# The last matrix product of an attention and two-layer kernel: half of its depth by seven quarter products per pair of tiles

## What is computed

```python
def _moe2_ref(x, w_in, w_out):      # x 1536x512, w_in 512x2048, w_out 2048x512
    h = x @ w_in
    r = np.maximum(h, 0.0)
    g = r * r
    return (g @ w_out).astype(np.float32)
```

## Time and profile before

| | before |
|---|---|
| median of 3 runs | 476.38 us (475.81 to 476.69) |
| the profiled execution | 474.66 us |
| its span | 472.9 us |
| mean granted TensorE clock over the span | 0.999 |
| PE, PEld, DVE, ACT, POOL busy | 98%, 84%, 64%, 45%, 27% |

### The profile page before, as it was taken

How to read it: one execution, slowest core, us unless ns; L and a number is a source line. 1 busy time by engine, 2 the same in 40 slices (tenths; PEclk the granted TensorE clock), 3 DMA queues, 4 the chain that set the end, 5 groups by cost and what they waited for, 6 DMA issues and landing times.

```text
span 472.9 us, 7375 instructions
## 1 busy us (share of the span) xinstructions
PE 462.9 (98%) x2754; PEld 395.4 (84%) x2754; DVE 303.9 (64%) x491; ACT 213.7 (45%) x538; POOL 126.0 (27%) x175
## 2 busy tenths in 40 slices
PE   8889999999999999999999999999999999999997
PEld 6667787887778887788999999999988888888885
DVE  3899888998898889874863766557974121212120
ACT  4687777656866576444554122222533212122210
POOL 2366333231311330512444576551000000000000
PEclk9999999999999999999999999999999999999999
DMA  7921124543564855464301111011511000000010
GB/s 225 326 85 48 52 71 138 169 126 78 162 169 130 189 134 156 110 152 117 91 1 46 44 46 46 0 44 49 191 73 45 23 22 24 22 24 22 22 46 22
DMA packets 60443, 41.87 MB, mean 89 GB/s; under 512 B 28344, under 2 KB 48056, under 8 KB 60408
## 3 DMA queue, kind: packets, MB, share of 16 engines
q1 hardware_dynamic: 59640, 40.74, 30.7%
q10 hardware_dynamic: 768, 0.66, 0.5%
HBM read 30.38 MB, written 11.01 MB: 88 GB/s over the span
## 4 chain that ended last, share of the span: by engine, by line
PE 90%; DVE 3%; POOL 3%; ACT 2%; issue 1%; DVEq 0%; POOLq 0%
PE wo_ps L1816 13%; PE h_ps L1776 12%; PE wt_ps L2031 9%; PE score_ps L2031 9%; PE score_ps L1978 7%; PE h_ps L2010 5%; PE score_ps L2010 5%; PE wo_ps L2031 5%; PE h_ps L2031 5%; PE wo_ps L2010 4%; PE wt_ps L2010 4%; PE wo_ps L1738 3%; PE score_ps L1704 3%; PE wt_ps L1704 1%; POOL pT_own L697 1%; PE wt_ps L1715 1%
## 5 line engine op out<-in xcount | busy, mean ns | idle before, releaser
L1573 DVE TENSOR_TENSOR g_lo<-g,g_hi 128x2048 fp32r<-128x2048 f32 (+2 forms) x14 | 27.7, 1986 | 76.4 <-ACT g_hi L1141 75.2
L1141 ACT ACTIVATE g_hi<-g 128x2048 fp32r<-128x2048 f32 (+2 forms) x14 | 23.3, 1671 | 84.9 <-PE score_ps L2031 25.2
L2031 PE MATMUL wt_ps<-wy,g_hi 128*128 128x512 f32 x128 | 39.7, 391 | 0.0
L2031 PE MATMUL score_ps<-wy,g_hi 128*128 128x512 f32 x128 | 39.7, 391 | 0.0
L882 ACT ACTIVATE prob<-sm,nbias 128x132 f32<-128x132 f32 (+1 forms) x96 | 37.7, 394 | 3.7 <-DVE nbias L1231 3.0
L1816 PE MATMUL wo_ps<-wo_hi,lnT_hi 128*128 128x512 f32 x88 | 36.1, 411 | 0.0
L1776 PE MATMUL h_ps<-w_hi,xT_hi 128*128 128x512 f32 x88 | 35.3, 401 | 0.8 <-DVE xT_lo L1340 0.5
L1816 PE MATMUL wo_ps<-wo_hi,lnT_lo 128*128 128x512 f32 x88 | 35.0, 398 | 0.0
L1776 PE MATMUL h_ps<-w_hi,xT_lo 128*128 128x512 f32 x88 | 34.5, 392 | 0.0
L1816 PE MATMUL wo_ps<-wo_lo,lnT_hi 128*128 128x512 f32 x88 | 34.4, 391 | 0.0
L1776 PE MATMUL h_ps<-w_lo,xT_hi 128*128 128x512 f32 x88 | 34.3, 390 | 0.0
(11 more groups left out here) (231 smaller groups left out, 1263.0 us busy)
## 6 DMA issues: line engine op xcount, KB each, us to landing
u_dram<-uT SPq DMA_DIRECT2D x18, 256.0 KB, 3.3
lnT_raw<-u_dram SPq DMA_DIRECT2D x36, 128.0 KB, 2.8
w_raw<-w_in SPq DMA_DIRECT2D x16, 256.0 KB, 3.3
V<-v SPq DMA_DIRECT2D x12, 256.0 KB, 3.3
wy_in<-w_out SPq DMA_DIRECT2D x6, 512.0 KB, 4.0
x_dram<-x SPq DMA_DIRECT2D x44, 64.0 KB, 2.2
out<-y SPq DMA_DIRECT2D x11, 256.0 KB, 2.0
k_raw<-kT SPq DMA_DIRECT2D x20, 132.0 KB, 2.8
```

What stands on the lines that cost most here:

```text
L1141: nc.scalar.activation(g_hi[t % 2][:, chunks, :], g_tile(t, chunks), ACT.Copy).then_inc(g_rounded, 1)
L1573: nc.vector.tensor_tensor(g_lo[t % 2][:, chunks, :], g_tile(t, chunks), g_hi[t % 2][:, chunks, :].bitcast(F32), ALU.subtract).then_inc(g_s ...
L2031: done = mm(y_ps[t % 8], gs[t % 2][:, n, :], wy[n // 2][:, n % 2, w, :], start=(n == 0 and k == 0), stop=(n == C2 - 1 and k == 2))
```

## The change

The second product works on pairs of tiles: pair p is the tiles p and p + 6. The depth is cut in two. The chunks of j = 0 to 3 (8 of 16) are multiplied plainly: 4 parts a pair, `plain_part(p, i)`, each with 4 chunks of one tile, 12 MATMULs of 512 columns. The chunks of j = 4 to 7 form a 2x2 problem, upper and lower tile by the rows r = 0 and 1 of the depth by the left and right 256 columns. It is made of seven products (`seven_part(p, i)`), each with 12 MATMULs of 256 columns. Their order is FIFTH, FIRST, THIRD, SIXTH, SECOND, SEVENTH, FOURTH. `PLAN` does the plain parts of three pairs, then the seven products of these pairs, and the same again for the other three.

Such a part or product is an item, 66 in all. ACT rounds an item (512 elements a row) into one of 7 ring slots (`RING`), and DVE subtracts in place (`g_low` is g's own memory). Item n + 7 is rounded once item n is done. For the seven products DVE also forms four sums of g per pair (S1 to S4, written over the pair's plain part of g, which is then used up) and, once, four differences of the quarters of w_out. These quarters are 7 operands of 1024 elements a row, each rounded and split once. THIRD, SECOND and FOURTH accumulate onto the plain result in PSUM (the last pair's FOURTH has a bank of its own, which DVE adds at the end by 256 columns). FIFTH has a bank of its own. FIRST, SIXTH and SEVENTH accumulate in one chain bank: ACT copies it after FIRST (`keep`), DVE reads it after SIXTH (`flush`), and both read it after SEVENTH.

```diff
-EARLY_TILES = 2
+PLAIN = 4
+RING = 7
+PLAN = (("plain", 0), ("plain", 1), ("plain", 2), ("seven", 0), ("seven", 1), ("seven", 2),
+        ("plain", 3), ("plain", 4), ("plain", 5), ("seven", 3), ("seven", 4), ("seven", 5))
+PAIR_PRODUCTS = ((S1, T1), (A11, B11), (S4, B22), (S2, T2), (A12, B21), (S3, T3), (A22, T4))
+FIFTH, FIRST, THIRD, SIXTH, SECOND, SEVENTH, FOURTH = range(NP)
...
+            def round_item(n):
+                kind, p, i = ITEMS[n]
+                if n < RING:
+                    act.wait_ge(multiplied, multiplied_before(NJ - 1) + (P_FIRST, P_SECOND, P_CORNER)[n // 3] + 1)
+                else:
+                    act.wait_ge(item_done, n - RING + 1)
...
+                nc.scalar.activation(item_high(n), item_raw(g, n), ACT.Copy).then_inc(item_rounded, 1)
...
+            for n in range(len(ITEMS)):
+                keep(n)
+                if n + RING < len(ITEMS):
+                    round_item(n + RING)
...
+            def prepare(n):
+
+                kind, p, i = ITEMS[n]
+                if kind == "seven" and i == FIFTH:
+                    sum_g(p, S1)
+                    sum_g(p, S2)
+                elif kind == "seven" and i == FIRST:
+                    sum_g(p, S3)
+                    sum_g(p, S4)
+                    dve.wait_ge(s_summed, len(WST_SUMS) * (p + 1))
+                split_item(n)
...
+                dve.wait_ge(item_done, n + 1)
+                if i == SIXTH:
+                    dve.wait_ge(kept, kept_before(p) + 1)
+                    nc.vector.tensor_tensor(upper[:, HALF:DM], chain_ps, lower[:, HALF:DM], ALU.add).then_inc(chain_summed, 1)
...
+            for n in range(len(ITEMS)):
+                flush(n)
+                if n + RING < len(ITEMS):
+                    prepare(n + RING)
+                if n == 1:
+                    sum_wst(T1)
+                    sum_wst(T2)
...
+                elif n == 7:
+                    split_wst(T4)
...
-                    for k in range(3):
-                        gs, w = ((g_hi, 0), (g_hi, 1), (g_lo, 0))[k]
-                        done = mm(y_ps[t % 8], gs[t % 2][:, n, :], wy[n // 2][:, n % 2, w, :],
-                                  start=(n == 0 and k == 0), stop=(n == C2 - 1 and k == 2))
...
+            def seven_part(p, i):
+
+                n = item("seven", p, i)
+                wk = PAIR_PRODUCTS[i][1]
+                pe.wait_ge(item_split, n + 1)
+                if p == 0:
+                    pe.wait_ge(wst_split, i + 1)
...
+                elif i == SIXTH:
+                    pe.wait_ge(kept, kept_before(p) + 2)
+                elif i == SEVENTH:
+                    pe.wait_ge(chain_summed, 2 * p + 1)
...
+                for c in range(NJ - PLAIN):
+                    for k in range(3):
+                        gs, w = ((item_high(n), 0), (item_high(n), 1), (item_raw(g_low, n), 0))[k]
+                        done = mm(bank, gs[:, c, :], wst[wk][:, w, c, :], start=((i in (FIFTH, FIRST) or bank is last_ps) and c == 0 and k == 0),
+                                  stop=(c == NJ - PLAIN - 1 and k == 2), skip_group_check=True)
```

More of the change, by code:

```diff
@@ L198, in gates_before, with parts_of, kept_before, item @@
     return len(BLOCKS) + 2 * (j - CLASSIC)
+def parts_of(kind):
+    return PARTS if kind == "plain" else NP
+ITEMS = tuple((kind, p, i) for kind, p in PLAN for i in range(parts_of(kind)))
+def kept_before(p):
+    return 3 * p
+def item(kind, p, i):
+    return ITEMS.index((kind, p, i))
 def seen(n):
@@ L641, in _ @@
                 load_wy(j)
[L642 to L646, removed]
-            sp.wait_ge(y_stored[1], 16 * (NT // 2 + 1))
+            for k in (B11, B22, B21, B12):
+                load_wst(k)
+            for p in range(NPAIR):
+                store_y(p, 0)
+                store_y(p, 1)
+            sp.wait_ge(y_stored[0], 16 * NPAIR)
+            sp.wait_ge(y_stored[1], 16 * (NPAIR + 1))
         def side_loads(act):
@@ new lines, in round_wst, with keep @@
+            def round_wst(k):
+                if k in WST_SUMS:
+                    act.wait_ge(wst_summed, WST_SUMS.index(k) + 1)
+                else:
+                    act.wait_ge(wst_loaded, 16 * 4)
+                nc.scalar.activation(wst[k][:, 0, :, :], wst_raw(k), ACT.Copy).then_inc(wst_rounded, 1)
+            def keep(n):
+                kind, p, i = ITEMS[n]
+                upper, lower = y[2 * (p % 2)], y[2 * (p % 2) + 1]
+                if kind == "plain" or i not in (FIFTH, FIRST, SEVENTH):
+                    return
+                act.wait_ge(item_done, n + 1)
+                if i == FIFTH:
+                    if p >= 2:
+                        act.wait_ge(y_stored[p % 2], 32 * (p // 2))
+                    nc.scalar.copy(lower[:, HALF:DM], fifth_ps).then_inc(kept, 1)
+                elif i == FIRST:
+                    nc.scalar.copy(upper[:, 0:HALF], chain_ps).then_inc(kept, 1)
+                else:
+                    nc.scalar.copy(lower[:, 0:HALF], chain_ps).then_inc(kept, 1)
@@ L1194, in _ @@
                 if j == NJ - 1:
-                    round_g(0, 0)
+                    for n in range(6):
+                        round_item(n)
                 corner(j)
@@ L1640, in _ @@
                 sum_3(j)
+                if last:
+                    split_item(2)
                 lower_right(j)
@@ L1646, in _ @@
                     split_wy(1)
-                    split_g(1, 0)
+                    split_item(3)
                     split_wy(2)
@@ L2047, in _ @@
                     multiply(j, n)
-            for first, last in ((0, 4), (4, 8), (8, C2)):
-                for t in range(EARLY_TILES):
-                    project2(t, first, last)
-            for t in range(EARLY_TILES, NT):
-                project2(t, 0, C2)
+            for kind, p in PLAN:
+                for i in range(parts_of(kind)):
+                    if kind == "plain":
+                        plain_part(p, i)
+                    else:
+                        seven_part(p, i)
 def kernel(q, k, v, n_sink, window, moe_w_in, moe_w_out, moe_g_ln, moe2_w_in, moe2_w_out):
```

266 lines of the change are left out of this document (181 added, 85 removed).

## The result

| | before | changed kernel |
|---|---|---|
| median of the runs beside each other | 476.1 us (475.58 to 476.69, 4 runs) | 470.79 us (470.05 to 471.9, 4 runs) |
| profiled execution, its span | 474.66, 472.9 | 471.22, 469.4 |
| second product, first to last MATMUL start | 131.65 | 126.91 |
| first MATMUL of the second product starts | 337.84 | 339.22 |
| last MATMUL start to the end of the span | 3.43 | 3.28 |

The ratio is 0.9892, with a 95% interval of 0.9873 to 0.9911: 5.3 us less, 4.2 to 6.0. A second set of runs, made later, gave 0.9912 (0.9884 to 0.994), about 4.2 us less; its profiled execution ran at a granted clock of 0.559 throughout (span 742.0 us), and its time is compared with none. The forecast was 6.65 us less, 469.7.

The account below looks back on a forecast made before the run. The second product was taken as bound by PE's MATMUL rate: 66.0 + 59.7 = 125.7 us against 131.9, 6.2 less, plus 0.45 at the end, 6.65 off, giving a median of 469.7 us, range 467.7 to 473.0.

Parts of the forecast that it names:

- the signs that it named: Blocks of 12 narrow MATMULs in 1.42 us, no idle PE, DVE about 85% busy, second product starting at 338.0.
- The count of the plain MATMULs: Second product: 288 MATMULs of 512 columns remain, at 0.2290 us each, 66.0 us.
- The narrow ones: Second product: 504 added MATMULs of 256 columns, at 0.1184 us each, 59.7 us.
- The rival on the weight load: Narrow MATMULs: full-height loads set the pace at 0.1737 us, costing 27.8 us more, 497.5; chance 6%.
- The reading of rows 6: Profile rows of weight loads: four loads of 96 rows, read as 0.11 us from each to the next.
- The end: After the last MATMUL: one add of 256 columns replaces two copies, and the last MATMUL is shorter, 0.45 us less.
- The handovers: Waits of SEVENTH for DVE's add and SIXTH for ACT's copy: spare 0.8 and 0.75 us, price 0.
- The first rival: Heavy pairs: DVE operations take 0.735 us, PE waits before SEVENTH, 1.9 us in all, 471.6; chance 15%.
- DVE's load: Pairs 0, 1, 3 and 4, where DVE also forms the next sums: 8.7 us of work in 9.95.
- The start: Before and early in the second product: added roundings hidden, DVE's first operands done at 366.8, needed at 371.0.
- late operands: Rival: w_out's quarters come late and PE stands once at 371, by 1 to 3 us, 471 to 473; chance 5%.
- bubbles at the 42 boundaries: Rival: small waits at the boundaries, at 0.15 us each 6.3 us, would leave no change; chance 4%.

Follow-up runs that it names:

- e10_places: e5_tail_spacer with operands of two plain chunks, and those of SECOND and SEVENTH, in other places; 469.71 us median, ratio 0.9875.
- e1: Changed kernel with the 504 narrow MATMULs streaming 192 of their 256 columns; one run, 467.66 us.
- e4: Changed kernel; in the last pair DVE takes out the lower plain result before SEVENTH and adds SEVENTH's sums without ACT's copy; one run, 469.98 us.
- e7: Changed kernel with sum S3 formed once more, waiting for its own result, in pairs that prepare another's sums; one run, 473.42 us.
- e3: Changed kernel with sum S3 formed twice more, each waiting for its own result, in pairs that prepare another's sums; 475.59 us median, ratio 1.0008.
- e6: Changed kernel with FOURTH's 12 MATMULs run once more per pair into FIFTH's idle bank; one run, 478.61 us.
- e5_tail_spacer: Changed kernel with e4's end and one extra MATMUL of 192 columns before the second group's plain parts; 469.8 us median, ratio 0.988.

## Why the prediction was right, and by how much not

It was right in direction and mechanism: the stage is bound by PE's pace, the narrow MATMULs are nearly half as long as the wide ones, and no wait takes the gain. It forecast 6.65 us and the trace shows 4.89 in the stage and behind it; the medians show 5.3 and 4.2. The measured 470.79 lies 1.1 above 469.7 and inside the range of 467.7 to 473.0. Of the signs that it named, the blocks took 1.44 us instead of 1.42, right at the pace of 0.12 above which it called itself wrong, DVE was busy for 92% of pair 1 instead of 85%, and the start was late by 1.37; no wait came back pair after pair.

**The count of the plain MATMULs** (66.0 us): 143 intervals of the first group took 32.73 us, 0.2289, as forecast. The second group took 33.37, 0.2333, which is 0.6 more. "288 x 0.2290" took for granted that a MATMUL's pace doesn't depend on what ran before.

**The narrow ones** (59.7 us): 0.1200 instead of 0.1184, 0.8 us more. The step that failed is the extrapolation "the step from 384 to 512 is 0.0553, and one further step down gives 0.1184". The 0.2290 from which it starts is a mean. In the kernel before, from the third tile on, the chunks of j = 6 and 7 came at 0.2267 and the others at 0.2288 to 0.2317. From 0.2267 to 0.1737 the step is 0.0530, and one more gives 0.1207. Put in another way, 0.2267 is 512 columns at 2.4 GHz (213.3 ns) and 13.4 ns; 0.1737 is 160.0 and 13.7; 0.1200 is 106.7 and 13.3. Columns and a gap of 13.3 to 13.7 ns fit these three. But it is a fit made afterwards, to the fastest of three paces at 512, and other rows don't lie on it: 0.118 for SECOND and SEVENTH in e10_places, a gap of 11.3, at most 0.1122 at 240 columns, and no gap at a granted clock of 0.559. What the gap consists of no run shows. In e10_places the forecast 0.1184 is even met by two products; that it wasn't met in the changed kernel hangs on the places of the operands too. The two terms, plain and narrow, explain the whole shortfall in the stage: 6.1 us were forecast from first to last MATMUL start, 4.74 came, and 0.8 + 0.6 is 1.4.

**Loads**: the rule of the loads that don't overlap is contradicted. A load is recorded as 192 ns long, the MATMULs follow at 120, all on the full height:

```profile
L2245 PEld LDWEIGHTS wo_ps<-wst,g_low 128*128 128x128 f32 x96 | 18.4, 192 | 0.0
```

The Trainium skill (TensorE: Matmul & The Clock Gate, Part 3, what overlaps and what doesn't) lets a load overlap matmuls in flight only with other row groups; 504 MATMULs here disagree. The same page of the Trainium skill (Part 2, Back-to-back issue gap) gives N/2.4 + 2.5 ns as the gap of matmuls on a warm array with no time for loads in it, by which an estimate for 256 columns is 0.109; the trace has 0.1200, where each MATMUL has a load of its own. The rival on the weight load did not come: its break-even was 0.132. The reading of rows 6, a pace of 0.11 below which a load with its MATMUL can't go, held: e1 found 0.1117 with full-height loads. That it is the load that sets this floor is likely but argued, since no run has narrow MATMULs without loads.

**The end** (-0.45): -0.15. Two things were wrong. "The first of the two copies took 0.34 before the second began, so 0.34 falls away" left out that the last add isn't alone. I placed 0.43 + 0.69 under FOURTH's 1.42 and forgot ACT's copy of 0.37 ahead of them and the 0.2 until SEVENTH's end is seen. From FOURTH's first MATMUL at 464.81 to the last add at 466.74 the chain took 1.93 us, while FOURTH's last MATMUL ended after 1.60. e4 shortens this chain, by ACT's copy and an add, and 0.47 is there. And the 0.11 of the shorter last MATMUL was counted twice, since the narrower slot of the last MATMUL is in the 6.2 already; the sum should have been 6.55.

**The handovers** (0.8 and 0.75 spare, price 0): the add before SEVENTH was done 0.57 before it in pair 1, and ACT's copy after FIRST at 385.70 for SIXTH at 386.57, 0.87. The price of 0 was right, the 0.8 was too much by half: the 0.15 until PE starts wasn't in it, so 0.42 is free. Counted from FOURTH's last MATMUL (issued at 382.13) the add ended after 6.75 us and not 6.3: DVE came to the flush 0.42 after that issue, not 0.19, and had four steps of 0.72 in front of the add, not two. (By the forecast's own count SEVENTH is issued at 7.22, not 7.10, since it starts one MATMUL after the last of SECOND; this hid 0.12 of the slip.) The first rival (DVE gives less than I count) did not come: the nine steps took 0.66 on the mean, waits included, where 0.735 would have made PE stand. But e7 and e3 show that its mechanism and its place were right: with one repeated sum more PE stands there pair after pair.

**DVE's load** (8.7 of 9.95): 9.28 of 10.10, more than forecast. Busy time counts each operation's own length, 0.68, where no other follows closely.

**The start**: the handover of the first operands was right. DVE finished what stands ahead of the sevens not at 366.8 but at 370.2, PE came at 372.18, and nothing waited:

```profile
369.01 1.22 DVE L1720 TENSOR_TENSOR wst<-wst_in,wst 128x1024 fp32r<-128x1024 f32 x1
370.14 1.89 DVE L1673 TENSOR_TENSOR g_low<-g,ring 128x512 fp32r<-128x512 f32 x3
```

Of the 4 us of spare that I counted, 2 were left. That the stage began at 339.38 on the chain and not 338.01 is none of the change's steps that I can find: 1.0 of the 1.37 us is there after the first 15 us, where PE waits for inputs, the rest comes before 200 us, and nine variants of the changed kernel, which do nothing else there, began at 338.5 to 340.4. But both traces of before began at 337.8 and 338.0. The medians speak for chance. An execution takes 1.7 to 1.8 us more than its span; less the stage and the end, the medians of before (475.13 to 476.1) leave an estimated start of the first MATMUL of 338.3 to 339.3, those of the changed kernel (470.79, 471.38) 338.8 and 339.4. So the two traced executions of before, at least 1.2 us below the medians of their sets, were early ones. A shift of some tenths is not excluded. The medians, 5.3 and 4.2 us apart, lie around the 4.89 that the traces give without it; that the first set came nearer to the forecast than that is chance.

**The other rivals**: late operands and bubbles at the 42 boundaries did not occur. 42 products of 12 took 1.44 us each, boundaries included, and e6 shows that 6 more do as well. The bubbles' price was 0. The first product's boundaries, from which I had argued it, told this rightly.

## What to carry to other kernels

When a stage is an unbroken row of MATMULs with a load each, price a width by its columns at the clock and the gap that neighbouring widths show (13 to 14 ns here, at a granted clock of 1.00) and not by a ratio: 256 columns took 0.1200 where 512 took 0.2290, and seven half-wide products for four wide ones give 8% of the time back instead of 12.5%. Such a gap is good to a nanosecond or two, one to two per cent of a narrow MATMUL. Follow each chain of handovers from the MATMUL that starts it, through every engine, to the one that needs it, the last one too: the chain with the one engine that I left out (ACT, 0.37 us) cost 0.32 of the gain at the end. Count such a chain to the start of the MATMUL that waits, not to the end of the one before: the 0.16 between them made 0.42 us of spare time look like 0.58. And before such a trick goes further (more levels, narrower pieces), look at both floors, here 0.112 us for a MATMUL with its load and 0.42 us of DVE's spare time.

## What the runs showed of the hardware

- A MATMUL of 512 columns, with a load each, came at 0.2267, 0.2289 or 0.2333 us in the same kernel at a granted clock of 1.00, by the place of its operands (e10_places) and by what ran before (e5_tail_spacer). 252 narrow MATMULs of 256 columns left the 143 intervals behind them at 0.2333; after one MATMUL of 192 columns, or when the narrow ones had 192 or 240 columns, they were at 0.2289 to 0.2292.
- MATMULs with a full-height load each follow each other at 0.1117 us with 192 columns and at 0.1117 to 0.1122 with 240, so the width doesn't count between these two. With 256 it is 0.1200, or 0.118 for two products whose operands were moved. A load is recorded as 188 to 192 ns long all the same.
- At a granted clock of 0.559 a MATMUL took 0.384 us with 512 columns and 0.192 with 256: half, with no gap to be seen.
- PE's first MATMUL starts 0.15 us after the DVE operation that it waits for has ended (eight times in e3 and e7).
- DVE operations of 512 elements a row, recorded as 0.68 to 0.69 us, start 0.60 or 0.72 apart (nine in pair 1 of the changed kernel).
